# Attention ahead of two gated layers: V products in two fp32r parts, nine score blocks for two heads, six narrow tiles mixed in

## What is computed

```python
# q, k, v: [4, 8, 576, 64]; tau: a scalar; moe_w_in, moe2_w_in: [512, 2048]; moe_w_out, moe2_w_out: [2048, 512]
scores = scale * np.matmul(q, k.transpose(0, 1, 3, 2))
thresh = np.max(scores, axis=-1, keepdims=True) - tau
scores = np.where(scores >= thresh, scores, -1000000000.0)
scores = scores - np.max(scores, axis=-1, keepdims=True)
attn = np.exp(scores)
attn = attn / (np.sum(attn, axis=-1, keepdims=True) + 1e-09)
attn_out = np.matmul(attn, v)
# tokens x 512, then two layers
h = x @ moe_w_in;  g = h * clip(h + 3, 0, 6) / 6;      x = g @ moe_w_out
h = x @ moe2_w_in; g = h / (1 + exp(-1.702 * h));      out = g @ moe2_w_out
```

## Time and profile before

| | before |
|---|---|
| median of 3 runs | 1230.28 us |
| span of the profiled execution (first to last instruction) | 1225.6 us |
| time of the runs less that span | 4.7 us |
| PE busy | 1184.3 us, 97% |
| DVE busy | 525.8 us, 43% |
| ACT busy | 563.2 us, 46% |
| POOL busy | 545.1 us, 44% |
| matmul records | 6408 |

### The profile page before, as it was taken

One profiled execution on the slowest core, in us unless ns is written; L12 is line 12 of the kernel. 1 busy time (PEld: TensorE's weight loads), 2 busy tenths in 40 slices (PEclk: granted clock), 3 DMA queues, 4 the chain that ended last, 5 costly groups with the idle time before them and its releaser, 6 DMA issues.

```text
span 1225.6 us, 19677 instructions
## 1 busy us (share of the span) xinstructions
PE 1184.3 (97%) x6408; PEld 1020.1 (83%) x6408; DVE 525.8 (43%) x1344; ACT 563.2 (46%) x1002; POOL 545.1 (44%) x457
## 2 busy tenths in 40 slices
PE   5999999989998999989999999999999999999998
PEld 3666677757776677789999999999999999999997
DVE  5777765576656766332222222222222322222221
ACT  5888765566645765444323333233333222222221
POOL 5888655456645565345333333224444222222222
PEclk9999999999999999999999999999999999999999
DMA  4333322141222312323233322112222112222210
GB/s 121 93 103 111 85 58 60 30 118 49 58 58 68 94 35 58 88 68 120 86 113 111 111 102 81 42 57 72 86 86 86 52 52 78 78 77 77 77 52 26
DMA packets 69736, 94.29 MB, mean 77 GB/s; under 512 B 24368, under 2 KB 45872, under 8 KB 69680
## 3 DMA queue, kind: packets, MB, share of 16 engines
q1 hardware_dynamic: 69680, 93.62, 24.8%
HBM read 70.01 MB, written 23.59 MB: 76 GB/s over the span
## 4 chain that ended last, share of the span: by engine, by line
PE 86%; DVE 4%; ACT 4%; issue 4%; POOL 0%; DMA 0%; DVEq 0%; ACTq 0%; SPq 0%; POOLq 0%
PE mm L417 19%; PE score L429 16%; PE tr L417 14%; PE score L427 12%; PE mm L403 10%; PE score L381 5%; PE tr L389 5%; PE mm L427 5%; ACT expd L663 2%; DVE neg_max L537 2%; DVE prob L551 1%; ACT w_hi L684 1%; ACT gate L702 1%; DVE act_f L580 1%; ACT x_hi L698 0%
## 5 line engine op out<-in xcount | busy, mean ns | idle before, releaser
L814 POOL TENSOR_TENSOR g_lo<-act_f,g_hi 128x384 fp32r<-128x384 f32 x192 | 193.8, 1014 | 442.8 <-ACT g_hi L710 442.8
L803 POOL TENSOR_TENSOR prob<-prob,inv_total 128x576 f32<-128x576 f32 x160 | 183.3, 1148 | 179.5 <-DVE inv_total L565 179.1
L403 PE MATMUL mm<-pt,v_raw 128*64 128x320 f32 (+1 forms) x640 | 182.4, 416 | 4.3 <-ACT o_t L678 4.3
L669 ACT ACTIVATE pt<-tr 128x640 f32<-128x640 f32 x160 | 112.3, 702 | 101.1 <-PE tr L389 100.1
L417 PE MATMUL mm<-x_hi,w_hi 128*128 128x384 f32 x432 | 149.6, 346 | 5.7 <-DVE x_lo L572 3.1
L551 DVE SCALAR_TENSOR_TENSOR prob<-score,thresh,expd 128x576 f32<-128x576 f32 x160 | 130.2, 813 | 50.4 <-ACT expd L663 43.7
L663 ACT ACTIVATE expd<-score,neg_max 128x576 f32<-128x576 f32 x161 | 118.9, 739 | 57.4 <-DVE neg_max L537 56.2
L417 PE MATMUL mm<-x_hi,w_lo 128*128 128x384 f32 x432 | 144.8, 335 | 0.0
L417 PE MATMUL mm<-x_lo,w_hi 128*128 128x384 f32 x432 | 144.7, 335 | 0.0
L537 DVE TENSOR_REDUCE neg_max<-score 128x1 f32<-128x576 f32 x161 | 121.5, 755 | 38.8 <-PE score L381 38.5
L403 PEld LDWEIGHTS mm<-pt,v_raw 128*64 128x64 f32 x640 | 77.1, 136 | 68.1 <-issue 22.0
(11 more groups left out here) (64 smaller groups left out, 2266.8 us busy)
## 6 DMA issues: line engine op xcount, KB each, us to landing
x_raw<-x_t_scratch SPq DMA_DIRECT2D x24, 768.0 KB, 5.8
q_raw<-in_qT SPq DMA_DIRECT2D x68, 144.0 KB, 2.8
k_raw<-in_kT SPq DMA_DIRECT2D x68, 144.0 KB, 2.9
stage<-in_w_in SPq DMA_DIRECT2D x16, 512.0 KB, 6.4
stage<-in_w_out SPq DMA_DIRECT2D x16, 512.0 KB, 6.5
x_t_scratch<-o_t SPq DMA_DIRECT2D x32, 144.0 KB, 2.4
part_t_scratch<-y_out SPq DMA_DIRECT2D x6, 768.0 KB, 4.2
part<-part_t_scratch SPq DMA_DIRECT2D x6, 768.0 KB, 7.8
```

Source lines behind the costliest of these rows:

```text
L403: m = pe.matmul(pv_out[0:HD, 0:n_q], v_raw[:, par, c, :], pt[:, c, cols], start=c == 0, stop=c == QB - 1)
L669: act.activation(pt[:, :, j * P:j * P + P], turned_p.rearrange("p (c n) -> p c n", c=QB), ACT.Copy).then_inc(pt_copied, 1)
L803: pool.tensor_tensor(p, p, inv_total[:, s % RING:s % RING + 1].broadcast_to([P, S]), ALU.mult).then_inc(norm_done, 1)
L814: pool.tensor_tensor(g_lo[:, c, :], act_f[:, c % 2, :], g_hi[:, c, :], ALU.subtract).then_inc(g_lo_done, 1)
```

## The change

The attention part is written anew, with no loops, and the order of all engines is laid out slot by slot in Python.

- The two heads of a pair share nine blocks instead of ten: four full blocks of each head and one block (`MID`, slot 4 of the pair) that holds the last 64 rows of both. Its scores are 8 matmuls, 4 for each head. There are 144 slots instead of 160.
- The transposed block is no longer copied as f32. ACT makes its high part `pt_hi` (`high_turned`), DVE subtracts that from PSUM and writes the low part `pt_lo` (`low_turned`); the list of blocks that POOL would do instead, `BY_POOL`, is empty. V is split into high and low columns side by side (`v_hl`, 128 columns). The product is then 5 matmuls with `pt_hi` in one slot and 5 with `pt_lo` in the next (`PV_HI`, `PV_LO`), in fp32r. Output rows 0 to 63 and 64 to 127 have to be added: ACT copies the lower half out (`copy_low_half`) and DVE adds (`merge`), in the slots that `MERGE` names.
- The threshold goes from DVE to POOL. Row sums are inverted once for two blocks. The exponent is written to `prob` and masked in place. POOL multiplies by the reciprocal with a tensor_scalar instead of a tensor_tensor with a broadcast operand.
- Step 0 of the layers has eight tiles of 288 tokens, and six of them (1728 tokens, not 1152) are mixed in: a piece of 12 matmuls in each of 8 of 9 slots (4 of 5 in the last batch), from slot 46 to slot 156. Two narrow tiles and 18 of 384 tokens remain behind attention.

The core of the diff:

```diff
-    SLOTS = 2 * QB
+    SLOTS = 2 * FULL + 1
+    MID = FULL
+    G = PAIRS * SLOTS
-    GROUPS = ((0, 2), (2, QB))
+    GROUP_COLS = ((0, 2 * P), (2 * P, 2 * P + TAIL), (0, TAIL + 2 * P), (TAIL + 2 * P, 2 * P))
+    PV_HI = {4: 0, 7: 1, 9: 2, 11: 3}
+    PV_LO = {5: 0, 8: 1, 10: 2, 12: 3}
+    MERGE = {6: 0, 9: 1, 11: 2, 13: 3}
+    BY_POOL = ()
-    TT = 384
-    TILES = NTOK // TT
+    NARROW, TT = HALF, 384
+    TILES = [(0, t * NARROW, NARROW) for t in range(NTOK // NARROW)]
+    TILES += [(step, t * TT, TT) for step in range(1, STEPS) for t in range(NTOK // TT)]
-    MIXED = B - 1
+    MIXED = 2 * (B - 1)
+    PIECES = 2 * FC
+    for b in range(1, B):
+        g0, every = BATCH_SLOTS * b + SLOTS + 1, 8 if b + 1 < B else 4
+        for p in range(2 * PIECES):
+            PIECE[g0 + p + p // every] = (2 * (b - 1) + p // PIECES, p % PIECES)
...
-                wait(pe, pt_copied, g)
+                        wait(pe, lo_by_dve, x - POOLED[x])
...
-                    wait(pe, pv_copied, 2 * head + group)
-                    m = pe.matmul(pv_out[0:HD, 0:n_q], v_raw[:, par, c, :], pt[:, c, cols],
-                                  start=c == 0, stop=c == QB - 1)
+            def prob_v(n, low):
+                if not low:
+                    pe.wait_ge(pt_hi_done, group_last(n) + 1)
+                    pe.wait_ge(v_lo_done, 2 * (n // 4) + side + 1)
+                    wait(pe, merged, n)
+                else:
+                    wait_low(pe, group_last(n))
+                for c in range(CHUNKS):
+                    p_part = (pt_hi, pt_lo)[low]
+                    m = pe.matmul(pv_out[:, 0:width], v_hl[:, side, c, :], p_part[:, GROUP_BUF[k], c, 0:width],
+                                  start=not low and c == 0, stop=low and c == CHUNKS - 1)
...
+            def low_turned(x):
+                dve.wait_ge(pt_hi_done, x + 1)
+                dve.tensor_tensor(pt_place(pt_lo, x), turned_place(x), pt_place(pt_hi, x), ALU.subtract
+                                  ).then_inc(lo_by_dve, 1)
+            def merge(n):
+                dve.tensor_tensor(o_t[:, n % 2, 0:width], pv_out[0:HD, 0:width], o_low[:, 0:width], ALU.add
+                                  ).then_inc(merged, 1)
...
+            for g in range(END):
+                done = PIECE.get(g - 1)
+                if g + 2 < G:
+                    row_max(g + 2)
+                if g + 1 < G:
+                    mask(g + 1)
+                    if (g + 1) % 2:
+                        invert((g + 1) // 2)
+                if 0 <= g - 2 < G and kind(g - 2) not in BY_POOL:
+                    low_turned(g - 2)
+                n = at_slot(MERGE, g)
+                if n is not None:
+                    merge(n)
```

More of the change, by code:

```diff
@@ L216, in tiles_of, with kind @@
[L216 to L239 removed]
+        def kind(x):
+            return x % SLOTS
@@ new lines, in pool_blocks, with wait_low, pt_place @@
+        def pool_blocks(x):
+            return sum(kind(y) in BY_POOL for y in range(x))
+        POOLED = [pool_blocks(x) for x in range(G + 1)]
+        def wait_low(eng, x):
+            wait(eng, lo_by_dve, x + 1 - POOLED[x + 1])
+            wait(eng, lo_by_pool, POOLED[x + 1])
+        def pt_place(tile, x):
+            s = kind(x)
+            if s != MID:
+                group, col = PLACE[s]
+                return tile[:, GROUP_BUF[group], :, col:col + P]
+            base = tile[:, 0, :, 2 * P:2 * P + TAIL]
+            after = tile[:, 1, :, 0:TAIL]
+            return bass.AP(tensor=base.tensor, offset=base.offset,
+                           ap=[list(base.ap[0]), list(base.ap[1]), [after.offset - base.offset, 2], list(base.ap[2])])
@@ L591, in drain_y @@
                 if partial is None:
-                    return dve.tensor_scalar(y_part(y_out, step, m), bank, scale, None, ALU.mult)
-                return dve.scalar_tensor_tensor(out=y_part(y_out, step, m), in0=bank, scalar=scale,
-                                                in1=y_part(part, step, m), op0=ALU.mult, op1=ALU.add)
-            def pair(i, unit, mlp):
-                for s in range(SLOTS):
-                    g = SLOTS * i + s
-                    mask(g, s)
-                    row_max(g + 1, s + 1)
-                    threshold(g + 1, s + 1)
-                    sum_total(g, s)
-                    if mlp is not None:
-                        mlp(s)
-                    invert(g, s)
@@ L621, in _ @@
-            attention(dve, pair, mix)
-            for k in range(KC):
-                low_x(MIXED, k)
-            def tile_body(step, tile, units):
-                base = first_item(step, tile)
+                    return dve.tensor_scalar(y_part(y_out, ti, m), bank, scale, None, ALU.mult)
+                return dve.scalar_tensor_tensor(out=y_part(y_out, ti, m), in0=bank, scalar=scale,
+                                                in1=y_part(part, ti, m), op0=ALU.mult, op1=ALU.add)
+            row_max(0)
@@ L835, in mix @@
[L835 to L848 removed]
+            low_q(0)
```

1018 lines of the change are left out of this document (540 added, 478 removed).

## The result

The changed kernel takes 1386.23 us (median of four runs, 1382.55 to 1386.41) against 1230.45 us for the kernel before (four runs, 1229.63 to 1230.89). The ratio is 1.1264, with a 95% interval of 1.1248 to 1.128. The change makes the kernel 156 us slower. The forecast was 1285 us, 1240 to 1320: the direction was right and the size was not, by 101 us.

What follows compares the result with a forecast made beforehand. PE was taken to bound the kernel, with attention already close to its pace. Start 16, unmixed slots 152, mixed 427, tail 30, narrow tiles 54, the rest 596 and 4.7 gave 1280, forecast 1285 us, range 1240 to 1320.

Steps and rivals of the forecast that it cites:

- What PE needs: PE's matmuls: 288 columns 0.133 us each, a mixed piece 1.60 us, some 94 us less work in all.
- The wait that the change adds: Attention: in three slots of nine PE stops before the high V product until merge is done, 2.85 us when mixed.
- The sum: Stage lengths from the start through attention, tail, narrow tiles and the rest, adding to 1280 us, so 1285 us measured.
- I cost the other edits at nothing: ACT's high part and copies, POOL's blocks and the threshold were taken to add no time.
- the 1170 us for the kernel without the wait: Whole-kernel time if merge does not hold PE: the sum less about 115 us.
- the 30 us of a pair: Attention pair's length, said to cover POOL's blocks even if each were a microsecond slower.
- the sum without waits: The stage lengths with PE's stops for merge taken out, about 115 us less, giving 1170 us.
- The span's ends: End of the kernel: 4.7 us to the span's end as now, and runs 4.7 us over the span.
- rival 2: The clock falls in unmixed attention pairs: 9 us a pair, 45 in all, 1300 to 1330 us; chance 0.12.
- rival 3: Attention: the wait as summed but in another size, 1262 to 1312 us; chance 0.78 together with the forecast.
- The bound of 1240: Whole kernel: lower end of the range, where half of the first rival's price would be gone.
- the first rival: Attention: VectorE's merge is not what holds PE, about 115 us less, 1170 us; chance 0.10.

Runs made afterwards that it cites:

- the middle merge: Changed kernel with only the merge moved ahead of the inversion and low part, and ScalarE's copy ahead of the exponent; 1328.44 us, ratio 1.0797.
- e11_both: Changed kernel with merge and copy first, tensor_tensor normalisation, single-column sums, k parts earlier and first-layer weight halves later; 1233.44 us, ratio 1.0031.
- the best version: e11_both with weight halves in the two narrow tiles moved behind the low parts or into the second tile; 1223.06 us, ratio 0.9938.
- e3_sum_single: Changed kernel with VectorE's two-column addition to the row sums made as two single-column instructions; 1374.83 us, ratio 1.1167.
- e2_norm_tt: Changed kernel with only GpSimd's normalisation put back to tensor_tensor with a broadcast operand; 1372.2 us, ratio 1.1145.
- e5_all_three: Changed kernel with merge and copy first in their slots, tensor_tensor normalisation and single-column sums; 1242.3 us, ratio 1.0095.
- e7_filler_all: Changed kernel with eight unused identity matmuls on PE before stopped products, in unmixed slots and mixed ones beginning a sum; 1361.95 us, ratio 1.1065.

## Why the prediction was wrong

**What PE needs** held. Narrow matmuls start 0.13 to 0.14 us apart at full clock, and a piece takes 1.59 us (forecast 1.60). Steps 1 to 3 take the 596 us of the earlier trace rows.

**The wait that the change adds** was right in place, number and length: 47 waits of 2.94 us, forecast 2.85 in mixed slots. The merge first in its slot gives 130 us back, the middle merge 58, the piece ahead of the product 73. The sum priced the waits at 115 us. The 130 include what the clock gave back, so the price was right to within that. At most 15 of the 101 us that are missing lie here, the other 86 in the kernel without the wait.

**"I cost the other edits at nothing"** is the step that failed, and with it the 1170 us for the kernel without the wait, on which the whole sum stood. The kernel with most of the wait gone measured 1256. Of the 86 us between, the runs brought back 33 (from 1256 to 1223). The parts don't add up simply, since each is worth something else beside the big wait than without it:

- GpSimd "at its present 1.15 us a block": it takes 1.77, because the change also replaced `tensor_tensor` by `tensor_scalar`, a line of the diff that I did not price apart from the row before. Worth 14 us in the changed kernel, nothing by itself once the wait is gone. I had set only the normalisation, 10.3 us, against "the 30 us of a pair". With all its parts GpSimd works 29.3 us in an unmixed pair, more than the 25.5 us that the pair has in the sum without waits. With `tensor_tensor` it works 23.7. The threshold, which I put at 0.2 us from VectorE, takes GpSimd 0.29.
- The inversion of two blocks at once, which I counted as half as many instructions: its sum lasts 0.47 us and up to 1.97, and stands in front of the low part and the merge. 11 us alone, 15 without the wait and beside `tensor_tensor`.
- GpSimd's low part of k, late in 15 waits (32 us of PE's time in the profile). Moved earlier, it gave 7 us without the wait, and 4 beside it (there together with the weight halves).
- The weight halves in the two narrow tiles: 62.8 us where I had put 54. I had added 3 us for them. Putting them elsewhere gave 10.
- The span's ends: 1.8 us between span and time here, not 4.7. The 4.7 set the span of one execution against the median of others: where the record has both for one execution of the kernel before, they are 2.1 to 2.2 us apart. 3 us the other way.

**The clock** was rival 2, limited to unmixed pairs, at 0.12 and 45 us. It fell to 0.82 there, and the small part of it that a run brought back was worth about 2 us. It also fell to 0.87 in the mixed stretch, where I had not looked for it, and cost some 20 at least. The reason that I gave against it, that the step stays at 0.133 through later waits, was read from waits of at most 1.6 us and a single one of 3.1 (at 524.8 us, with the clock at 1.00 before and after); here PE stood nearly 3 us at a time, three slots in nine. The mean of the first product's 288-column matmuls in the mixed bank fits: in the changed kernel the group L444 with `x_lo` has 331 ns, in `e11_both`, at a clock of 0.97 in that stretch, 295. The Trainium skill, page "TensorE: Matmul & The Clock Gate", section "HAM oscillation — how this bites in real kernels", says that waits between bursts bring the clock down again and again. The trace agrees: the level changes within a single piece, behind a wait of 2.37 us. The waits of that section's example are longer than those here.

**Slips in the working** that did not move the forecast: rival 3's own terms (10 less, 20 more, 0 to 12 for ACT) give 1275 to 1317 us, not 1262 to 1312. The bound of 1240 is where half of the 91 us of mixed waits would be gone; half of the first rival's 115 would be 1228. The two narrow tiles at 54 us take 46 us out of the later work, not 48.

**What stays open** is 53 us, the distance from 1223 to 1170. By stage, 27 of them lie ahead of the first mixed piece (174.2 us in the best version, 147 in the sum without waits) and 30 in the mixed stretch; the tiles and the ends take 4 back. Unmixed pairs return after 30.4 us there, where the sum without waits had 25.5 (30.3 less three times 1.6), and mixed ones after 34.3, where it had 30.8. The rows of `e11_both` point to ScalarE's list (51.9 us of waits of the merge for its copy). I had called it free because its copies lie "in slots of 3.6 us and more". That is the length of a mixed slot; an unmixed one has 2.6 us in the same sum, and in the stretch shown above ScalarE works without a gap from 102.39 to 105.79 us, 3.4 us, on what one slot gives it (high part, exponent, q and k) before the copy. It has time enough over a pair (20.3 us of work), but not at the moment at which VectorE needs the copy. No run shortened that list, and the one that moved the merge away from it was slower, so this cause is argued, not shown. A rival stands beside it untested: in the best version the granted clock is still 0.87 from 50 to 160 us, while PE stands and starts there for short work.

## What to carry to other kernels

A wait summed from the rows can be right to a few per cent and the forecast still be off by 100 us, if the same kernel without the wait is taken from an ideal count. Price that case first: all the work of each engine in a stretch against the length that the sum gives it, and every changed form of instruction in it, even where an engine seems to have room. In engines that work down a fixed list, put first what another engine stands for, and put ahead of a wait whatever doesn't need it: here five moves in the lists and two forms of instruction turned 12.6% slower into 0.6% faster with no change in the arithmetic.

## What the runs showed of the hardware

- GpSimd multiplies 128x576 by a per-partition factor in 1.77 us as `tensor_scalar` and in 1.16 us as `tensor_tensor` with the factor broadcast. The Trainium skill, page "GPSIMD Engine Reference", section "Engine selection", has it the other way round: one-input work at roughly line rate, two-input work about twice as slow as on VectorE. The measurement decides: here the form with one tensor input and a factor is the slower one.
- VectorE's addition of a constant takes 143 to 156 ns on one column whatever GpSimd does (`e3_sum_single`). On two columns it takes 168 to 171 ns when GpSimd is idle, and up to 1974 ns beside it in the changed kernel: where it starts during a `tensor_tensor` of GpSimd it ends, in nearly every case, 0.02 to 0.03 us behind that instruction. Beside GpSimd's `tensor_scalar` of 128x576 it was held less, and five of twelve ran in 168 to 170 ns. The Trainium skill names a mechanism (page "VectorE: DVE Perf Modes", section "What auto-detection actually checks": a two-port mode for a single source and a destination in SBUF whose outermost sizes are both even or equal; page "GPSIMD Engine Reference", section "Key points": such instructions contend with GpSimd for the SBUF interfaces that both share). The trace agrees for two columns. One column is equal on both sides as well, and is not held in the runs; there the measurement decides.
- `x_lo`, which subtracts two tiles in SBUF, grew on 288 columns from 702 ns in the changed kernel to 953 in `e2_norm_tt`, where nothing but GpSimd's normalisation changed (to two inputs), and to 1006 in `e5_all_three`. The shortest take 443 ns. So the faster form on GpSimd has a price on VectorE.
- The granted clock was 0.87 from 200 to 700 us with stops of PE of 2 to 3 us in three of nine slots, 0.93 with matmuls that compute nothing in part of the stops (`e7_filler_all`), and 0.97 with most of the stops gone (`e11_both`). Its two levels show as starts 0.24 and 0.14 us apart for 288 columns.
